# Products of 64 rows on two row tiles in the last 16 units of a three-stage kernel

## The chip, the cores and the metric

The kernel runs on one core of a Trainium2 chip. The metric is the device time of one execution in microseconds (us). The engines are TensorE (PE; its weight loads are listed apart, as PEld), VectorE (DVE), ScalarE (ACT), GpSimd (POOL) and the DMA queues, of which SyncE (SP) issues nearly all.

## What is computed

Three stages follow one another over 8192 tokens of 192 channels: a causal convolution of 7 taps, and two expansions to 2048 features and back. The first has a rational function between its products, the second a squared ReLU.

```python
out = np.einsum('hk,bskhg->bshg', w, x_unf)      # 7 taps, weights after a softmax

h = x @ w_in                                      # layer 1: 192 -> 2048
P = a[0] + a[1] * h + a[2] * h2 + a[3] * h3
Q = 1.0 + np.abs(b[0]) * np.abs(h) + np.abs(b[1]) * h2
g = P / (Q + 1e-06)
x = g @ w_out                                     # 2048 -> 192

h = x @ w_in                                      # layer 2: 192 -> 2048
r = np.maximum(h, 0.0)
g = s * (r * r) + b
out = g @ w_out                                   # 2048 -> 192
```

## The kernel before

The tokens are cut into 16 tiles of 512. The 2048 features are 16 blocks of 128, and a unit is two blocks of one tile, so there are 128 units, 8 to a tile. Every engine runs its own instruction stream over units `n` in order; streams meet only at semaphores. A loop holds tiles 2 to 13. Tiles 0 and 1, tiles 14 and 15 (units 112 to 127) and two tiles' worth of steps behind them are written out, so that `n` is a plain integer there. Layer 2 works on unit `m = n - 10` while layer 1 works on unit `n`.

In each unit TensorE issues four groups, in this order:

- the first product of layer 1 (L403 to L410), ten matmuls of 512 columns with type float32r: for each of the two blocks (`half`), the high and the low part of `x` by the high weights, the high part by the low weights, and two products with the 64 remaining channels. The tail tile `x_tail` holds the high part of those 64 channels in one half of its rows and the low part in the other; `w1_tail_hi` and `w1_tail_lo` hold their 64 rows twice. Block 0 goes to one PSUM bank of `h1`, block 1 to the other. The last matmul raises `h1_ready`.
- the second product of layer 2 for unit `m - 1` (`second_product_2`, L450 to L469): 8 float32 matmuls of 192 columns, each of which TensorE carries out as two weight loads and two matmuls (16 records in the trace), into two banks of `o2`. Where it is the tile's last (`k == UNITS - 1`) the order is by bank.
- the first product of layer 2 for unit `m` (L430 to L448), again ten matmuls of 512 columns, into the two banks of `h2`. For the first unit of a tile it waits for the parts of its input as they come: `x2_hi_ready`, `x2_lo_ready`, and the tail's two.
- the second product of layer 1 for unit `n - 2` (`second_product_1`, L412 to L428), ten matmuls of 512 columns. Six wait for `gh_ready` (ScalarE), four for `gl_ready` (GpSimd).

All matmuls use all 128 rows of the array. Each has its own weight load. `h1` has a single buffer: the first product of layer 1 waits for `t3_done` of the unit before (L539), which VectorE raises at L887 after ScalarE's L667 and L668 and its own L881 and L884. ScalarE's further steps are L672 to L721. VectorE's for the quotient are L905 to L911, and GpSimd makes the low part of `g` at L394. At step `j == 2` of a tile the results `o1` and `o1_tail` are split into the input of layer 2 (ACT L686 and L688, DVE L838 to L851).

Of the kernel before, what the change touches and what calls it, by code (L numbers as in the profile page):

```python
# [5 lines left out]
P = 128  # L6
TOK = 512
# [18 lines left out]
def conv_rational_relu2_kernel(nc, x_main, x_tail, weight, w_in1, w_out1, a, b, w_in2, w_out2, s, b2, out):  # L26
# [4 lines left out]
    D, FF = w_in1.shape  # L31
    TAIL = D - P
    FT = FF // P
    UNITS = FT // 2
# [3 lines left out]
    NU = TILES * UNITS  # L38
# [5 lines left out]
    OUT2_LAG = 1  # L44
# [31 lines left out]
    with ExitStack() as ctx:  # L76
# [6 lines left out]
        def sem(name):  # L83
            return ctx.enter_context(nc.semaphore(name))
# [3 lines left out]
        w1_hi = sb("w1_hi", [P, FF], F32R)  # L88
        w1_lo = sb("w1_lo", [P, FF], F32R)
        w1_tail_hi = sb("w1_tail_hi", [P, FF], F32R)  # L90
        w1_tail_lo = sb("w1_tail_lo", [P, FF], F32R)
# [103 lines left out]
        x2_lo_ready, x2_sum_ready = sem("x2_lo_ready"), sem("x2_sum_ready")  # L195
        x2_tail_hi_ready, x2_tail_lo_ready = sem("x2_tail_hi_ready"), sem("x2_tail_lo_ready")
        y_ready_out = sem("y_ready_out")

# [18 lines left out]
        def in_h2(n):  # L219

            return isinstance(n, int) and n < SKEW and n % 2 == 1
# [13 lines left out]
        def late_exponential(n):  # L235

            return not isinstance(n, int) or n > SKEW

        def is_end(n):
            return isinstance(n, int) and n == NU  # L240
# [159 lines left out]
        def _(pe):  # L400
            def first_product_of_layer_1(h, k, x_hi, x_lo, x_tail):

                for half in range(2):  # L403
                    c = slice((2 * k + half) * P, (2 * k + half + 1) * P)
                    pe.matmul(h[:, half, :], w1_hi[:, c], x_hi[:, :], start=True, stop=False)  # L405
                    pe.matmul(h[:, half, :], w1_hi[:, c], x_lo[:, :], start=False, stop=False)  # L406
                    pe.matmul(h[:, half, :], w1_lo[:, c], x_hi[:, :], start=False, stop=False)  # L407
                    pe.matmul(h[:, half, :], w1_tail_hi[:, c], x_tail[:, :], start=False, stop=False)  # L408
                    last = pe.matmul(h[:, half, :], w1_tail_lo[:, c], x_tail[:, :], start=False, stop=True)  # L409
                last.then_inc(h1_ready, 1)  # L410

            def second_product_1(n, k, buf):  # L412
                pe.wait_ge(gh_ready, counted(n - OUT1_LAG + 1))
                for half in range(2):
                    f = 2 * k + half
                    c = slice(half * TOK, (half + 1) * TOK)
                    tail = v1_tail[:, f].rearrange("p a b -> p (a b)")
                    pe.matmul(o1[:, :], v1_hi[:, f, :], gh[:, buf, c], start=(f == 0), stop=False)  # L418
                    pe.matmul(o1[:, :], v1_lo[:, f, :], gh[:, buf, c], start=False, stop=False)  # L419
                    pe.matmul(o1_tail[:, :], tail, gh[:, buf, c], start=(f == 0), stop=False)  # L420
                pe.wait_ge(gl_ready, counted(n - OUT1_LAG + 1))
                for half in range(2):
                    f = 2 * k + half
                    c = slice(half * TOK, (half + 1) * TOK)
                    tail = v1_tail[:, f].rearrange("p a b -> p (a b)")
                    pe.matmul(o1[:, :], v1_hi[:, f, :], gl[:, buf, c], start=False, stop=(f == FT - 1))  # L426
                    last = pe.matmul(o1_tail[:, :], tail, gl[:, buf, c], start=False, stop=(f == FT - 1))  # L427
                last.then_inc(out1_done, 1)  # L428
# [21 lines left out]
            def second_product_2(k, buf):  # L450
                def product(half, c):
                    f = 2 * k + half
                    g = g2[buf][:, half * TOK + c * P:half * TOK + (c + 1) * P]
                    return pe.matmul(o2[:, c // 2, c % 2, 0:D], g, v2[:, f, :],  # L454
                                     start=(f == 0 and c % 2 == 0), stop=(f == FT - 1), skip_group_check=True)

                if k == UNITS - 1:

                    for bank in range(2):
                        for half in range(2):  # L460
                            for c in (2 * bank, 2 * bank + 1):
                                last = product(half, c)
                        if bank == 0:
                            last.then_inc(out2_half_done, 1)
                else:
                    for half in range(2):
                        for c in range(SUB):
                            last = product(half, c)
                last.then_inc(out2_done, 1)  # L469
# [57 lines left out]
            def product_of_layer_1(n, j, t, parity):  # L527

                if j == 0:
                    pe.wait_ge(x1_hi_ready, counted((t + 1) * 2))  # L530
                    pe.wait_ge(x1_lo_ready, counted((t + 1) * 2))
                if first(t) and j in (1, 2, 4, 6):

                    high, low = {1: (2, 4), 2: (4, 6), 4: (10, 9), 6: (10, 10)}[j]
                    pe.wait_ge(w_hi_ready, high)
                    pe.wait_ge(w_lo_ready, low)

                two_buffers = isinstance(n, int) and n <= SKEW
                pe.wait_ge(t3_done, counted(n - 1 if two_buffers else n))  # L539
                first_product_of_layer_1(h2 if in_h2(n) else h1, j, x1_hi[parity], x1_lo[parity], x1_tail[parity])  # L540

            def second_product_of_layer_1(n, j, t):
                k = (j - OUT1_LAG) % UNITS
# [8 lines left out]
            def second_product_of_layer_2(t, j, m, k2):  # L552

                if unit(m - OUT2_LAG):
                    k = (k2 - OUT2_LAG) % UNITS
                    if k == 0:

                        tk = t + (j - SKEW - OUT2_LAG) // UNITS
                        pe.wait_ge(y_ready_out, counted(tk * 2))
                        pe.wait_ge(conv_copied, 4)  # L560
                        pe.wait_ge(v2_loaded, 16)
                    pe.wait_ge(g2_ready, counted(m - OUT2_LAG + 1))
                    second_product_2(k, (j - OUT2_LAG) % 2)

            def phase(n0, t, i, parity):
                for j in range(UNITS):
                    n, m = n0 + j, n0 + (j - SKEW)
                    k2 = (j - SKEW) % UNITS
                    t2 = t + (j - SKEW) // UNITS

                    early = isinstance(n, int) and n < SKEW
                    if unit(n) and not (isinstance(n, int) and n <= SKEW):
                        product_of_layer_1(n, j, t, parity)
                    if early and n == 0:
                        first_product_of_first_unit()
                    if early:
                        product_of_layer_1(n + 1, (n + 1) % UNITS, (n + 1) // UNITS, (n + 1) // UNITS % 2)

                    if tile(t):
                        second_product_of_layer_2(t, j, m, k2)  # L580
                    if j == 3 and first(t):
                        pe.wait_ge(ones_ready, 1)
                        pe.wait_ge(v2_loaded, 16)
                        for f in range(FT):
                            last = pe.matmul(o2[:, 0, 0, 0:D], ones, v2[:, f, :], start=(f == 0),
                                             stop=(f == FT - 1))
                        last.then_inc(colsum_ready, 1)
                    if early:
                        conv_of_unit(n)
                    if unit(m):  # L590
                        if k2 == 0:
                            pe.wait_ge(w_hi_ready, 13)
                            pe.wait_ge(w_lo_ready, 14)
                        if isinstance(m, int) and m == UNITS // 2:

                            pe.wait_ge(w_hi_ready, 14)
                            pe.wait_ge(w_lo_ready, 18)
                        pe.wait_ge(u_ready, counted(m))
                        if in_h2(n - 1):
                            pe.wait_ge(t3_done, n)  # L600
                        x2p = (parity + (j - SKEW) // UNITS) % 2
                        first_product_of_layer_2(k2, x2p, t2)

                    ends_layer_1 = not tile(t) and j == OUT1_LAG - 1
                    if not tile(t) and not ends_layer_1:
                        second_product_of_layer_2(t, j, m, k2)
                    if unit(n - OUT1_LAG):
                        second_product_of_layer_1(n, j, t)
                    if ends_layer_1:
                        second_product_of_layer_2(t, j, m, k2)  # L610
# [353 lines left out]
```

## Time and profile before

| | |
|---|---|
| median of the runs | 1266.53 us (2 runs, 1266.32 to 1266.73) |
| profiled execution, its own time | 1267.56 us |
| its span, first to last instruction | 1265.7 us |
| TensorE, matmuls | 1250.9 us busy, 99% of the span, 6018 records |
| TensorE, weight loads | 1078.0 us busy, 6018 records |
| VectorE | 1119.9 us |
| ScalarE | 1073.1 us |
| GpSimd | 331.4 us |
| mean granted TensorE clock | 0.997 of full speed |

The rows quoted further on have the forms of the page and of the trace's views. In the timeline a row is start, duration (both us), engine, line of the kernel, operation, output and inputs, and how often in a row; square brackets hold the idle time before it and what ended it. A matmul's duration in the trace is a modelled latency: matmuls overlap, and the time that one adds is the distance from one start to the next.

### The profile page before, as it was taken

The numbers are of one execution on the slowest core, as the hardware profiler recorded it, in microseconds if no ns is written. First come the engines' busy times: TensorE is split into PE (matmuls) and PEld (weight loads), VectorE is DVE, ScalarE is ACT, GpSimd is POOL, SyncE is SP. The second block draws the span as 40 slices with busy tenths as digits, with TensorE's granted clock in tenths as the row PEclk, the third lists the DMA queues.
The fourth block names the chain that finished last, engine by engine and source line by source line (L and its number), as shares of the span: only waits on it lengthen the run. The fifth ranks groups of instructions, "written<-read, shape, count | busy, mean of one in ns | idle before, by whom it ended". The sixth has DMA issues, their size and how long they took to land.

```text
span 1265.7 us, 16270 instructions
## 1 busy us (share of the span) xinstructions
PE 1250.9 (99%) x6018; PEld 1078.0 (85%) x6018; DVE 1119.9 (88%) x1031; ACT 1073.1 (85%) x1091; POOL 331.4 (26%) x153
## 2 busy tenths in 40 slices
PE   7999999999999999999999999999999999999999
PEld 5767888888888888888888888888888888888888
DVE  7997999998999989998999989999899998888740
ACT  6898888988989888888888889898898888888853
POOL 3443222322222222223223222222232232222210
PEclk8999999999999999999999999999999999999999
DMA  7100000010000100000000100001000000000000
GB/s 223 61 10 17 1 13 1 1 39 0 12 0 12 25 0 12 0 12 25 11 1 0 38 0 12 0 0 38 0 12 0 12 0 1 13 1 13 1 13 13
DMA packets 14748, 20.39 MB, mean 16 GB/s; under 512 B 1792, under 2 KB 9984, under 8 KB 14592
## 3 DMA queue, kind: packets, MB, share of 16 engines
q1 hardware_dynamic: 14576, 20.01, 5.4%
q8 instruction: 18, 0.29, 0.1%
q14 instruction: 10, 0.08, 0.0%
q10 hardware_dynamic: 144, 0.01, 0.0%
HBM read 13.72 MB, written 6.29 MB: 16 GB/s over the span
## 4 chain that ended last, share of the span: by engine, by line
PE 90%; DVE 6%; issue 1%; DMA 1%; ACT 1%; SPq 1%; POOL 0%; DVEq 0%; ACTq 0%
PE o L454 26%; PE h L436 5%; PE h L437 5%; PE h L441 4%; PE h L446 4%; PE h L447 4%; PE o L426 4%; PE h L405 4%; PE h L409 4%; PE o_tail L427 4%; PE h L407 4%; PE h L406 4%; PE h L408 4%; PE o_tail L420 4%; PE o L419 4%; PE o L418 4%
## 5 line engine op out<-in xcount | busy, mean ns | idle before, releaser
L394 POOL TENSOR_TENSOR gl<-work,gh 128x1024 fp32r<-128x1024 f32 x128 | 309.5, 2418 | 830.0 <-ACT gh L677 822.6
L454 PE MATMUL o<-v,work 128*128 128x192 f32 x2048 | 353.3, 326 | 0.9 <-issue 0.9
L454 PEld LDWEIGHTS o<-v,work 128*128 128x128 f32 x2048 | 339.1, 190 | 11.1 <-issue 1.3
L667 ACT ACTIVATE work<-h,coef 128x1024 f32<-128x1024 f32 x128 | 154.3, 1205 | 135.1 <-PE h L409 134.3
L881 DVE SCALAR_TENSOR_TENSOR work<-work,coef,h 128x1024 f32<-128x1024 f32 x128 | 163.8, 1280 | 74.8 <-ACT work L668 72.4
L911 DVE SCALAR_TENSOR_TENSOR work<-work,coef 128x1024 f32<-128x1024 f32 x128 | 164.5, 1285 | 4.5
L887 DVE SCALAR_TENSOR_TENSOR work<-work,coef,h 128x1024 f32<-128x1024 f32 x128 | 164.0, 1281 | 4.5
L905 DVE SCALAR_TENSOR_TENSOR work<-work,coef 128x1024 f32<-128x1024 f32 x128 | 164.1, 1282 | 0.0
L907 DVE SCALAR_TENSOR_TENSOR work<-work 128x1024 f32<-128x1024 f32 x128 | 159.0, 1242 | 4.4
L884 DVE TENSOR_TENSOR work<-work,h 128x1024 f32<-128x1024 f32 x128 | 155.4, 1214 | 0.0
L710 ACT ACTIVATE work<-h 128x1024 f32<-128x1024 f32 x128 | 130.3, 1018 | 23.9 <-PE h L447 23.8
L721 ACT ACTIVATE work<-work,coef 128x1024 f32<-128x1024 f32 x128 | 145.6, 1137 | 0.0
L668 ACT ACTIVATE work<-h,coef 128x1024 f32<-128x1024 f32 x128 | 141.3, 1104 | 0.0
L677 ACT CAST gh<-work 128x1024 fp32r<-128x1024 f32 x128 | 133.9, 1046 | 8.5 <-DVE work L911 8.3
L713 ACT ACTIVATE work<-work 128x1024 f32<-128x1024 f32 x128 | 136.0, 1063 | 4.5
L706 ACT ACTIVATE work<-work 128x1024 f32<-128x1024 f32 x128 | 134.8, 1053 | 2.9 <-DVE work L881 2.8
L672 ACT ACTIVATE work<-work 128x1024 f32<-128x1024 f32 x128 | 136.5, 1066 | 0.1
L436 PE MATMUL h<-x_hi,w_hi 128*128 128x512 f32 x256 | 117.4, 459 | 2.0 <-ACT x_hi L686 2.0
L405 PE MATMUL h<-x_hi,w_hi 128*128 128x512 f32 x254 | 99.9, 393 | 4.1 <-ACT w_tail_hi L624 4.0
L418 PE MATMUL o<-gh,v_hi 128*128 128x512 f32 x256 | 102.8, 402 | 0.0
L426 PE MATMUL o<-gl,v_hi 128*128 128x512 f32 x256 | 100.0, 391 | 0.9 <-POOL gl L394 0.8
L446 PE MATMUL h<-x_tail,w_tail_hi 128*128 128x512 f32 x256 | 99.7, 389 | 0.9 <-DVE x_tail L851 0.9
(101 smaller groups left out, 2015.3 us busy)
## 6 DMA issues: line engine op xcount, KB each, us to landing
out_dram<-y_out SPq DMA_DIRECT2D x32, 192.0 KB, 2.0
xt<-in_x_main_dram SPq DMA_DIRECT2D x7, 518.0 KB, 5.0
xt_tail<-in_x_tail_dram SPq DMA_DIRECT2D x8, 259.0 KB, 5.3
work<-in_moe_w_out_dram SPq DMA_DIRECT2D x2, 768.0 KB, 8.6
v<-in_moe_w_out_dram SPq DMA_DIRECT2D x1, 1536.0 KB, 6.2
raw_w_tail_late<-in_moe_w_in_dram SPq DMA_DIRECT2D x4, 256.0 KB, 7.1
work<-in_moe_w_in_dram SPq DMA_DIRECT2D x2, 512.0 KB, 5.7
xt<-in_x_main_dram SPq DMA_DIRECT2D x2, 259.0 KB, 7.6
```

What stands on the lines that cost most here:

```text
L394: nc.gpsimd.tensor_tensor(gl[:, j % 2, :], r_buf[j % 2], gh[:, j % 2, :].bitcast(F32), ALU.subtract).then_inc(gl_ready, 1)
L418: pe.matmul(o1[:, :], v1_hi[:, f, :], gh[:, buf, c], start=(f == 0), stop=False)
L426: pe.matmul(o1[:, :], v1_hi[:, f, :], gl[:, buf, c], start=False, stop=(f == FT - 1))
L436: pe.matmul(h2[:, half, :], w2_hi[:, c[half]], x2_hi[x2p][:, :], start=True, stop=False)
L454: return pe.matmul(o2[:, c // 2, c % 2, 0:D], g, v2[:, f, :], start=(f == 0 and c % 2 == 0), stop=(f == FT - 1), skip_group_check=True)
L667: nc.scalar.activation(t_of_n, h_flat, ACT.Identity, bias=a2, scale=a3).then_inc(t_ready, 1)
L881: nc.vector.scalar_tensor_tensor(q_buf[buf], w_of_n, b0_abs, h_flat, ALU.add, ALU.mult).then_inc(z_done, 1)
L884: nc.vector.tensor_tensor(t_of_n, t_of_n, h_flat, ALU.mult).then_inc(t2_done, 1)
L887: nc.vector.scalar_tensor_tensor(num_buf[buf], t_of_n, a1, h_flat, ALU.add, ALU.mult).then_inc(t3_done, 1)
L905: nc.vector.scalar_tensor_tensor(q, q, one_eps, r, ALU.add, ALU.mult).then_inc(e_done, 1)
L907: nc.vector.scalar_tensor_tensor(r, q, 2.0, r, ALU.subtract, ALU.mult, reverse0=True).then_inc(r1_done, 1)
L911: nc.vector.scalar_tensor_tensor(r, num, a0, r, ALU.add, ALU.mult).then_inc(g_ready, 1)
```

## The change

The diff adds three predicates. In units 112 to 127 (`rows_1`) the first product of layer 1, and in units `n` = 116 to 127 (`rows_2`) the first product of layer 2, is made by `by_rows`. In units 120 to 127 (`rows_3`), except where `k == UNITS - 1`, the second product of layer 2 is made by `second_product_2_by_rows`.

`by_rows` cuts each matmul into one over rows 0 to 63 (`LOWER`) and one over rows 64 to 127 (`UPPER`). It goes in two turns: in the first, block 0 takes the lower rows and block 1 the upper rows, alternating; in the second it is the other way round. Between the turns TensorE waits for its own matmuls of the first turn (`turned`), since both row tiles would otherwise write one bank. Of the product with `w_tail_lo` only the rows `high` are made, those that hold the high part of `x`; the product of two low parts falls away. `second_product_2_by_rows` does the same with the two banks of `o2`.

```diff
+        def rows_1(n):
+            return isinstance(n, int) and NU - 2 * UNITS <= n < NU
+
+        def rows_2(n):
+            return rows_1(n) and n >= NU - 2 * UNITS + UNITS // 2
+
+        def rows_3(n):
+            return rows_1(n) and n >= NU - UNITS
...
+            LOWER, UPPER = slice(0, P // 2), slice(P // 2, P)
+            turns = [0]
+
+            def turn_over():
+
+                turns[0] += 2
+                pe.wait_ge(turned, turns[0])
+
+            def by_rows(h, k, products, tail_low, high, done):
+
+                c = [slice((2 * k + half) * P, (2 * k + half + 1) * P) for half in range(2)]
+                for turn in range(2):
+                    for weights, x, ready in products:
+                        if turn == 0 and ready is not None:
+                            pe.wait_ge(*ready)
+                        for half in range(2):
+                            rows = (LOWER, UPPER)[(half + turn) % 2]
+                            last = pe.matmul(h[:, half, :], weights[rows, c[half]], x[rows, :],
+                                             start=turn == 0 and weights is products[0][0] and x is products[0][1],
+                                             stop=turn == 1 and weights is products[-1][0] and rows != high)
+                            if turn == 0 and weights is products[-1][0] and rows != high:
+                                last.then_inc(turned, 1)
+                    weights, x = tail_low
+                    half = turn if high == LOWER else 1 - turn
+                    last = pe.matmul(h[:, half, :], weights[high, c[half]], x[high, :], start=False, stop=turn == 1)
+                    if turn == 0:
+                        last.then_inc(turned, 1)
+                        turn_over()
+                last.then_inc(done, 1)
+
+            def first_product_of_layer_1_by_rows(h, k, x_hi, x_lo, x_tail, high):
+                by_rows(h, k, ((w1_hi, x_hi, None), (w1_hi, x_lo, None), (w1_lo, x_hi, None), (w1_tail_hi, x_tail, None)),
+                        (w1_tail_lo, x_tail), high, h1_ready)
+
+            def first_product_of_layer_2_by_rows(k, x2p, t2):
+                of_x = [(x2_hi_ready, t2 + 1), (x2_lo_ready, t2 + 1), (x2_tail_lo_ready, t2 + 1)] if k == 0 else [None] * 3
+                by_rows(h2, k, ((w2_hi, x2_hi[x2p], of_x[0]), (w2_lo, x2_hi[x2p], None), (w2_hi, x2_lo[x2p], of_x[1]),
+                                (w2_tail_hi, x2_tail[x2p], of_x[2])), (w2_tail_lo, x2_tail[x2p]), LOWER, h2_ready)
+
+            def second_product_2_by_rows(k, buf):
+                for turn in range(2):
+                    for half in range(2):
+                        f = 2 * k + half
+                        for c in range(2):
+                            for bank in range(2):
+                                rows = (LOWER, UPPER)[(bank + turn) % 2]
+                                col = half * TOK + (2 * bank + c) * P
+                                last = pe.matmul(o2[:, bank, c, 0:D], g2[buf][rows, col:col + P], v2[rows, f, :],
+                                                 start=(f == 0 and c == 0 and turn == 0), stop=(f == FT - 1 and turn == 1),
+                                                 skip_group_check=True)
+                                if turn == 0 and half == 1 and c == 1:
+                                    last.then_inc(turned, 1)
+                    if turn == 0:
+                        turn_over()
+                last.then_inc(out2_done, 1)
...
+                if rows_1(n):
+                    first_product_of_layer_1_by_rows(h1, j, x1_hi[parity], x1_lo[parity], x1_tail[parity],
+                                                     tail_rows[parity])
...
+                    if isinstance(t, int) and rows_3(t * UNITS + j) and k != UNITS - 1:
+                        second_product_2_by_rows(k, (j - OUT2_LAG) % 2)
...
+                        if rows_2(n):
+                            first_product_of_layer_2_by_rows(k2, x2p, t2)
```

## Rows read from the trace of the kernel before

**Rows 1.** The page, engines' busy time, and granted clock in 40 slices
```profile
PE 1250.9 (99%) x6018; PEld 1078.0 (85%) x6018; DVE 1119.9 (88%) x1031; ACT 1073.1 (85%) x1091; POOL 331.4 (26%) x153
...
PEclk8999999999999999999999999999999999999999
```
**Rows 2.** Busy time by stretch: matmuls, loads, DVE, ACT, POOL, clock, DMA
```profile
1054.20:1091.80 37.60, 37.60 (x186) 32.85 (x185) 34.93 (x35) 33.31 (x35) 9.69 (x4) 1.00 0.04 12
1167.00:1204.70 37.70, 37.70 (x186) 32.98 (x185) 29.65 (x25) 32.32 (x33) 9.69 (x4) 1.00 0.00 0
1204.70:1235.00 30.30, 29.36 (x148) 25.40 (x148) 12.41 (x12) 15.68 (x17) 4.78 (x2) 1.00 0.04 14
```
**Rows 3.** Timeline of unit 118, TensorE and who frees h1
```profile
1110.61 0.39 PE L405 MATMUL h<-x_hi,w_hi 128*128 128x512 f32 x1
1110.61 0.19 PEld L406 LDWEIGHTS h<-x_lo,w_hi 128*128 128x128 f32 x1
...
1112.65 0.39 PE L409 MATMUL h<-x_tail,w_tail_lo 128*128 128x512 f32 x1
1112.65 2.69 PEld L454 LDWEIGHTS o<-v,work 128*128 128x128 f32 x16
1112.88 2.76 PE L454 MATMUL o<-v,work 128*128 128x192 f32 x16
1113.13 1.20 ACT L667 ACTIVATE work<-h,coef 128x1024 f32<-128x1024 f32 x1 [1.31 <-PE h L409]
...
1115.47 0.19 PEld L437 LDWEIGHTS h<-x_hi,w_lo 128*128 128x128 f32 x1
...
1117.75 0.39 PE L418 MATMUL o<-gh,v_hi 128*128 128x512 f32 x1
1117.89 1.28 DVE L887 SCALAR_TENSOR_TENSOR work<-work,coef,h 128x1024 f32<-128x1024 f32 x1
...
1120.02 0.39 PE L405 MATMUL h<-x_hi,w_hi 128*128 128x512 f32 x1
```
**Rows 4.** Timeline where TensorE waits for ScalarE, behind unit 127
```profile
1213.66 1.05 ACT L677 CAST gh<-work 128x1024 fp32r<-128x1024 f32 x1 [2.89 <-DVE work L911]
...
1214.40 0.39 PE L447 MATMUL h<-x_tail,w_tail_lo 128*128 128x512 f32 x1
1214.76 0.19 PEld L418 LDWEIGHTS o<-gh,v_hi 128*128 128x128 f32 x1 [0.39 <-ACT gh L677]
1214.76 0.50 PE L418 MATMUL o<-gh,v_hi 128*128 128x512 f32 x1
...
1214.87 0.19 PEld L419 LDWEIGHTS o<-gh,v_lo 128*128 128x128 f32 x1
1215.09 0.40 PE L419 MATMUL o<-gh,v_lo 128*128 128x512 f32 x1
```
**Rows 5.** Timeline of unit 122, where layer 2 takes a new tile
```profile
1152.87 0.69 DVE L851 TENSOR_TENSOR x_tail<-x_sum,x_tail 64x512 fp32r<-64x512 f32 x1
...
1152.99 0.53 PE L436 MATMUL h<-x_hi,w_hi 128*128 128x512 f32 x1
1153.13 0.19 PEld L437 LDWEIGHTS h<-x_hi,w_lo 128*128 128x128 f32 x1
```
**Rows 6.** Timeline, TensorE's other waits for layer 1's last units
```profile
1211.28 0.19 PEld L426 LDWEIGHTS o<-gl,v_hi 128*128 128x128 f32 x1 [0.56 <-POOL gl L394]
...
1217.22 0.19 PEld L426 LDWEIGHTS o<-gl,v_hi 128*128 128x128 f32 x1 [1.23 <-POOL gl L394]
```

More of the change, by code:

```diff
@@ L197, in conv_rational_relu2_kernel @@
         y_ready_out = sem("y_ready_out")
+        turned = sem("turned")
         W2_HALF = [slice(0, FF // 2), slice(FF // 2, FF)]
@@ L539, in product_of_layer_1 @@
                 pe.wait_ge(t3_done, counted(n - 1 if two_buffers else n))
-                first_product_of_layer_1(h2 if in_h2(n) else h1, j, x1_hi[parity], x1_lo[parity], x1_tail[parity])
+                if rows_1(n):
+                    first_product_of_layer_1_by_rows(h1, j, x1_hi[parity], x1_lo[parity], x1_tail[parity],
+                                                     tail_rows[parity])
+                else:
+                    first_product_of_layer_1(h2 if in_h2(n) else h1, j, x1_hi[parity], x1_lo[parity], x1_tail[parity])
             def second_product_of_layer_1(n, j, t):
@@ L562, in second_product_of_layer_2 @@
                     pe.wait_ge(g2_ready, counted(m - OUT2_LAG + 1))
-                    second_product_2(k, (j - OUT2_LAG) % 2)
+                    if isinstance(t, int) and rows_3(t * UNITS + j) and k != UNITS - 1:
+                        second_product_2_by_rows(k, (j - OUT2_LAG) % 2)
+                    else:
+                        second_product_2(k, (j - OUT2_LAG) % 2)
             def phase(n0, t, i, parity):
@@ L601, in phase @@
                         x2p = (parity + (j - SKEW) // UNITS) % 2
-                        first_product_of_layer_2(k2, x2p, t2)
+                        if rows_2(n):
+                            first_product_of_layer_2_by_rows(k2, x2p, t2)
+                        else:
+                            first_product_of_layer_2(k2, x2p, t2)
                     ends_layer_1 = not tile(t) and j == OUT1_LAG - 1
```

## The prediction

> **What bounds the kernel now.** I read the page first, for which engine fills the span. Matmuls are busy 1250.9 of 1265.7 us, and the granted clock stays at its upper level in 39 of 40 slices [rows 1]. The busy time by stretch says whether this holds where the change works. In the four units from 1054.20 and in the four up to 1204.70 TensorE is busy in every microsecond, and only the stretch behind them (1204.70 to 1235.00) has 0.94 us of gaps [rows 2]. The timeline of one unit then gives the price of each instruction. From one L405 to the next unit's is 1120.02 - 1110.61 = 9.41 us [rows 3]. The ten products of 512 columns from L418 at 1117.75 to 1120.02 take 2.27 us, 0.227 each. The 16 records of L454 run from 1112.88 to the start of the next stream (when the load of L437 begins, 1115.47), 2.59 us or 0.162 each. 30 x 0.227 + 16 x 0.162 = 9.40 us, so a unit is its matmuls and nothing else: what TensorE gains or loses in units 112 to 127 is a gain or loss of the whole, nearly one to one.
>
> How much it could gain before another engine stops it: `h1` is free when L887 ends, 1117.89 + 1.28 = 1119.17, and the next L405 starts at 1120.02 [rows 3]. Slack exists, but it is 0.6 to 0.85 us a unit, and a slower TensorE widens it.
>
> **The streams: nothing removed.** Ten full matmuls become 18 half ones, which looks like nine. But a turn has five half products on the row tile that `high` names and four on the other. The wait between the turns keeps the idle tile from going on. So the path is 2 turns x 5 streams = 10 streams of 512 columns, as before. If two row tiles do run side by side and a half-height stream takes 0.227 as a full one does, the saving is 0. A bound on the gain side is the float32 rows: 0.162 us for 192 columns in two cycles each is 0.422 ns a column-cycle, or 0.216 for 512 [rows 3]. By that rate it would be 28 products x 10 x 0.011 = 3.1 us. I take 0.
>
> **The wait between turns: added, 35 times.** There are 28 products by rows (16 of layer 1 and 12 of layer 2) and 7 second products of layer 2 (units 120 to 127 without 122). The wait can't be answered before the last matmul has written, and the next load stands behind the wait. Nothing else is in that engine's queue, so nothing hides it. Three pieces. A matmul's record lasts 0.39 us where the next one starts 0.23 after it, so 0.16 is not covered [rows 3]. From ScalarE's end at 1213.66 + 1.05 = 1214.71 to the load that waited for it (1214.76) is 0.05. That load keeps the matmul waiting until 1214.87, 0.11 more [rows 4]. 0.16 + 0.05 + 0.11 = 0.32, and 35 x 0.32 = 11.2 us. Lower bound 0.16 (the load passes the wait): 5.6. Upper bound: from a last matmul's modelled end, 1112.65 + 0.39, to the start of the ScalarE instruction that waited for it, 1113.13, are 0.09 [rows 3]; in place of 0.05 that gives 0.36, 12.6 us.
>
> **The second tile starts late: 28 times.** In each turn the second tile's load can begin only when the first one's is done, 0.11 later [rows 4]. In one of a product's two turns `high` is the second tile, and its five streams end 0.11 after 5 x 0.227. 28 x 0.11 = 3.1 us; the lower bound is 0, if both load at once. Further on, two loads take 0.22 in a pair's 0.227, which just fits.
>
> **The second product of layer 2: loads become the limit.** Its weights are `g2`, new in every matmul. 16 records become 32, each with a load. At 0.11 a load that is 3.52 us where the streams need 16 x 0.162 = 2.59: +0.93 in each of 7 units, 6.5 us. In the rows every load begins as the matmul before it starts [rows 3]. If that holds over two tiles too, the order A, A, B, B of the two passes gives 2 x (0.162 + 0.11) = 0.544 for four records, 8 x 0.544 = 4.35 us, +1.76 a unit and 12.3 us in all. The other end is 0 (two tiles load side by side). I take 6.5, which rests on the measured load alone.
>
> **Changing between 128 and 64 rows.** No row of before shows such a change. There are 42: two in each of units 112 to 115, four in 116 to 119, two in the seven units where all three groups are by rows, four in unit 122 (8 + 16 + 14 + 4). The lower end is 0: a load of float32 weights into a float32r stretch starts on time, at 1112.65 [rows 3]. The upper end is a full drain and a load behind it, 0.16 + 0.11 = 0.27, or 11.3 us. I take the drain alone, 0.16 x 42 = 6.7 us. The Trainium skill has a rule that speaks against this change ("TensorEngine Tiling (Array Packing)", Key Properties): changing the tiling mode drains the engine. With the rule the 6.7 stands or becomes 11.3; without it the term is 0. No row here shows it.
>
> **What takes some back, what costs nothing.** Behind unit 127 TensorE waits 0.56, 0.39 and 1.23 us for layer 1's last elementwise chain [rows 4, 6]. In unit 127 the slower groups after its layer 1 product add about 1.25 (second product) + 0.6 (first product of layer 2), and that chain runs on meanwhile: -1.5 us, between -2.2 and 0. The reordered waits of unit 122 cost nothing. The tail is ready at 1152.87 + 0.69 = 1153.56, while the stream starts at 1153.13 and comes to the tail after three pairs, at 1153.81 [rows 5]. The `h1` loop grows with the product itself and stays under the longer unit. The 28 x 8 + 7 x 16 = 336 more matmul records and their loads are fetched beside the work.
>
> **Sum:** 11.2 + 3.1 + 6.5 + 6.7 - 1.5 = +26.0 us on the profiled 1267.6, or 1293.6. The median of the runs is 1.0 lower, so **1293 us**, +2.1%. With every term at its lower bound (5.6 - 2.2 - 3.1) it is about 0, with every term at its upper one (12.6 + 3.1 + 12.3 + 11.3) +39. With only the second products and the change of height at 0 it is 11.2 + 3.1 - 1.5 = +12.8. Own range: 1279 (+12.8) to 1306 (+39).
>
> **Rivals.**
>
> *A, no overlap.* The row tiles don't run side by side, so the change does not do what it says. 8 more streams in 28 products, 224 x 0.227 = 50.8 us, and 16 more records in 7 units, 112 x 0.162 = 18.1 us. With the turns and switches (11.2 + 6.7 - 1.5) that is +85, 1352 us. For it: no row of before shows two matmuls in the array. Against: the tiles share neither rows nor banks. The skill has a measured gain of 3.07 for four row tiles of 32 rows ("TensorE: Matmul & The Clock Gate", Measured speedup vs the span model); no run here shows it.
>
> *B, loads don't hide under a matmul of their own rows.* Each stream then costs its load as well, 0.227 + 0.11 = 0.337. A turn is 5 x 0.11 = 0.55 longer, 56 turns 30.8 us; the second products go to 16 x (0.162 + 0.11) = 4.35, +12.3. With 11.2 + 3.1 + 6.7 - 1.5 it is +63, 1329 us. The skill has the rule that loads overlap matmuls in flight only where the row group differs (same page, The mechanism). The trace speaks against it for full-height matmuls: the load of L406 begins with the matmul of L405 at 1110.61, and the next starts 0.227 later [rows 3]. It may hold for tiles.
>
> *C, not slower by what can be measured.* The two tiles load weights side by side and across a change of height, so nothing of the load side is new: stagger, second products and switches all 0. Only the turns are left, 11.2 - 1.5 = +9.7, 1276 us. It decides from where those three terms (16.3 here) fall below some 15. For it: the rows bound them below by 0. Against: the load is a single record stream at 0.11 apiece.
>
> *D, the clock.* Shorter bursts with gaps of a third of a us could let the granted clock fall to its lower level. A unit at 1.2 GHz costs nearly twice 9.4, so a few of them would be +20 us and more. Against: gaps of 0.56 and 1.23 us leave the clock at 1.00 in that stretch [rows 2, 6].
>
> **Chances.** The forecast with its own range 0.67, A 0.10, B 0.11, C 0.10, D 0.02. The range leaves out A and D and the lower part of C and takes in B: 1277 to 1330. Some 2% (25 us) is what can be told from no change, and my sum lies at that edge. Of the forecast's 0.67, 0.35 lies above it and 0.32 below. Slower by over 2%: 0.35 + 0.10 + 0.11 + 0.02 = 0.58. Within 2%: 0.32 + 0.09 = 0.41. Faster by over 2% is 0.01: the 280 streams by rows (63.6 us) would have to be 40% shorter, at no cost for the turns.
>
> **What would show it.** The new products as 64-row records, block 0 and block 1 starting 0.11 apart and each tile's next 0.227 later (right) or 0.227 and 0.454 (A), 0.337 (B). A gap of 0.55 from a turn's last start to the next turn's first matmul. The distance from L454's last record to the first half-height one near 0.33 (drain) or 0.16 (none). Second products by rows of 3.5 + 0.3 us. Units 112 to 115 at about 10.2 us, 120 to 127 at about 12. I am wrong if a tile's stream is far from 0.227, or if a change of height costs more than a turn.

## The result, and the profile after

| | before | after |
|---|---|---|
| median of the runs | 1266.53 us | 1287.85 us (2 runs, 1287.76 to 1287.93) |
| profiled execution, its span | 1267.56, 1265.7 us | 1287.76, 1285.9 us |
| matmul records | 6018 | 6354 |
| VectorE, ScalarE busy | 1119.9, 1073.1 us | 1119.8, 1074.4 us |

The changed kernel takes 1.0167 of the time before, with a 95% interval of 1.0147 to 1.0187. That is 21.3 us more by the medians and 20.2 us by the spans of the two profiles. The number foretold was 1293, the range 1277 to 1330.

In the page of the changed kernel the other engines do the same work as before [rows 1]. The granted clock (one digit a slice, in tenths) stays at its upper level from the first slice to the last:

```profile
PE 1270.8 (99%) x6354; PEld 1074.4 (84%) x6354; DVE 1119.8 (87%) x1031; ACT 1074.4 (84%) x1091; POOL 330.7 (26%) x153
...
PEclk9999999999999999999999999999999999999999
```

The 19.9 us more of matmul "busy" time are not all work, since a matmul's record is a latency. Where the time sits is seen in the timeline of the changed kernel's first unit by rows, 112 (start, duration, engine, line, operation, how many; in brackets the idle time before it and what ended it). L441 and L448 are `by_rows`, L522 is the full-height second product of layer 2:

```profile
1054.06 0.20 PEld L441 LDWEIGHTS h<-x_hi,w_lo 64*128 64x128 f32 x2
1054.29 0.40 PE L441 MATMUL h<-x_hi,w_lo 64*128 64x512 f32 x2
1054.29 0.20 PEld L441 LDWEIGHTS h<-x_tail,w_tail_hi 64*128 64x128 f32 x2
1054.52 0.40 PE L441 MATMUL h<-x_tail,w_tail_hi 64*128 64x512 f32 x2
1054.53 0.18 PEld L448 LDWEIGHTS h<-x_tail,w_tail_lo 64*128 64x128 f32 x1
1054.76 0.38 PE L448 MATMUL h<-x_tail,w_tail_lo 64*128 64x512 f32 x1
1055.20 0.19 PEld L441 LDWEIGHTS h<-x_hi,w_hi 64*128 64x128 f32 x2 [0.49 <-PE h L448]
...
1055.31 0.19 PEld L441 LDWEIGHTS h<-x_lo,w_hi 64*128 64x128 f32 x2
...
1056.24 0.39 PE L448 MATMUL h<-x_tail,w_tail_lo 64*128 64x512 f32 x1
...
1056.56 2.57 PEld L522 LDWEIGHTS o<-v,work 128*128 128x128 f32 x16 [0.37 <-issue]
```

Three things are to be read here.

- Two half-height matmuls start together: a pair is one line of 0.40 us, and the next pair starts 0.23 us after it, where full-height matmuls stand 0.227 apart [rows 3]. Their two weight loads go together too: both fit in 0.20 us, where one takes 0.19.
- The turn: the last stream of turn 1 starts at 1054.76, the next load at 1055.20 and its stream at 1055.31, where the load after it starts. That is 0.55 in place of 0.23, so the turn (the point where TensorE waits for its own matmuls) costs 0.32.
- The change of height: from the last short stream at 1056.24 to the load of the next full one at 1056.56 are 0.32, and 0.11 more to its stream. That is 0.43 in place of 0.23, so a change costs 0.20. Its releaser is "issue": the profile shows nothing that is waited for.

The change in the other direction costs as much, 1063.60 to 1063.92 to 1064.03 at the start of unit 113:

```profile
1063.60 0.39 PE L495 MATMUL o_tail<-gl,v_tail 128*128 128x512 f32 x1
...
1063.92 0.19 PEld L441 LDWEIGHTS h<-x_hi,w_hi 64*128 64x128 f32 x2 [0.35 <-issue]
...
1064.03 0.19 PEld L441 LDWEIGHTS h<-x_lo,w_hi 64*128 64x128 f32 x2
```

So unit 112 takes 1053.83 to 1064.03 between the first streams of its layer 1 products, 10.20 us against 9.41 [rows 3]: one turn (0.32), two changes (0.40), and 0.07 for streams a little further apart (four distances in 0.93 us from 1053.83, 0.233 each, in place of 0.227). In the last tile, where all three groups are by rows, a unit takes 10.93 us (1193.27 to 1204.20), and there the full-height streams of L486 to L495 stand 0.231 apart as well. Whatever spaces the streams out is therefore not the half height alone.

What TensorE's loads waited for from unit 112 on, in the changed kernel (us in total, times, longest):

```profile
PEld h L441 <- PE h L448: 13.6, 28, 0.5
PEld h L441 <- issue: 6.5, 20, 0.4
...
PEld o L486 <- issue: 4.4, 12, 0.4
PEld o L522 <- issue: 3.3, 9, 0.4
PEld o L471 <- PE o L471: 2.5, 7, 0.4
...
PEld o L494 <- POOL gl L406: 1.0, 1, 1.0
```

28 + 7 = 35 waits of TensorE for itself, as counted. Of the 42 changes of height, 41 show here as idle time ended by "issue" (20, 12 and 9); the first, into unit 112 at 1053.72, lies before this window. The last row is the wait for layer 1's chain behind unit 127, which was 2.18 us in three places before [rows 4, 6].

### The profile page after: what moved, and what is told of

Its sections match the earlier page's. It is cut to its first block, busy times and chain, and to the rows that moved or that the text cites. A ratio compares the mean times of both kernels' runs of the same rounds, so it can differ in the third digit from the quotient of the medians.

```text
span 1285.9 us, 16941 instructions
## 1 busy us (share of the span) xinstructions
PE 1270.8 (99%) x6354; PEld 1074.4 (84%) x6354; DVE 1119.8 (87%) x1031; ACT 1074.4 (84%) x1091; POOL 330.7 (26%) x153
## 4 chain that ended last, share of the span: by engine, by line
PE 90%; DVE 6%; issue 1%; DMA 1%; ACT 1%; SPq 0%; POOL 0%; DVEq 0%; ACTq 0%
PE o L522 24%; PE h L441 5%; PE o L486 4%; PE o L494 4%; PE o_tail L495 4%; PE o_tail L488 4%; PE o L487 4%; PE h L514 4%; PE h L504 4%; PE h L515 4%; PE h L505 4%; PE h L509 4%; PE h L418 4%; PE h L421 4%; PE h L420 4%; PE h L419 4%
## 5 line engine op out<-in xcount | busy, mean ns | idle before, releaser
L522 PE MATMUL o<-v,work 128*128 128x192 f32 x1936 | 335.0, 326 | 0.6 <-issue 0.6
L522 PEld LDWEIGHTS o<-v,work 128*128 128x128 f32 x1936 | 319.9, 190 | 12.9 <-issue 4.3
L504 PE MATMUL h<-x_hi,w_hi 128*128 128x512 f32 x232 | 106.5, 459 | 2.5 <-ACT x_hi L764 2.5
L486 PE MATMUL o<-gh,v_hi 128*128 128x512 f32 x256 | 104.1, 407 | 0.0
L488 PE MATMUL o_tail<-gh,v_tail 128*128 128x512 f32 x256 | 99.8, 390 | 0.0
L487 PE MATMUL o<-gh,v_lo 128*128 128x512 f32 x256 | 99.8, 390 | 0.0
```

Source lines behind the costliest of these rows:

```text
L504: pe.matmul(h2[:, half, :], w2_hi[:, c[half]], x2_hi[x2p][:, :], start=True, stop=False)
```

## The experiments

Theory T, formed on this profile: 35 turns at 0.32 us and 42 changes of height at 0.20 us make 19.6 us of the 21.3, and the streams and loads add next to nothing. Rival S: half-height matmuls side by side slow one another down. The experiments take away each cost alone, or put it alone into the kernel before. All times are beside runs of the kernel before on the same chip. Numbers in brackets behind a ratio are its 95% interval. Where two changed kernels are compared, it is by their medians; the kernel before has medians of 1266.53 to 1267.09 us from set to set, so such a difference holds to about 0.5 us.

### The turn taken away

```diff
-                            rows = (LOWER, UPPER)[(half + turn) % 2]
+                            rows = (LOWER, UPPER)[half]
...
-                    half = turn if high == LOWER else 1 - turn
+                    half = 0 if high == LOWER else 1
...
-                    if turn == 0:
-                        last.then_inc(turned, 1)
-                        turn_over()
```

(and the same in `second_product_2_by_rows`)

> The changed kernel, but in the second turn each block stays on the row tile it had in the first, so the wait between the turns falls away (the products of the other row halves are left out, and the same halves are made twice: as many matmuls, in as many streams). Theory T (the loss is 35 waits for TensorE's own matmuls at 0.32 us each and 42 changes between 128 and 64 rows at 0.20 us each, all else near 0): 11.2 us less than the changed kernel, about 1276.6 us. Rival S (half-height matmuls side by side are themselves slower, by contention of their streams or loads): stays near 1287.

Measured: 1273.92 us beside 1266.64, ratio 1.0056 (1.0040 to 1.0073), +7.3 us. The waits were worth 13.9 us here, 2.7 more than 35 x 0.32. The trace shows from where. In this kernel without waits, at the end of a second product (L466), one row tile already loads the next group's weights (L441) while the other tile is not done:

```profile
1138.07 0.19 PEld L441 LDWEIGHTS h<-x_hi,w_hi 64*128 64x128 f32 x1
1138.21 0.19 PEld L466 LDWEIGHTS o<-v,work 64*128 64x128 f32 x1
1138.23 0.19 PEld L441 LDWEIGHTS h<-x_hi,w_lo 64*128 64x128 f32 x1
1138.37 0.19 PEld L466 LDWEIGHTS o<-v,work 64*128 64x128 f32 x1
1138.46 0.18 PEld L441 LDWEIGHTS h<-x_lo,w_hi 64*128 64x128 f32 x1
```

The tile that has four streams in a turn where the other has five doesn't stand idle any more but goes ahead. A unit of the last tile takes 9.51 us here (1133.78 to 1143.29) with two changes of height in it, so by subtraction 9.11 without them, under the 9.41 of full height. Two things come together for this that only the last tile has. All three groups there are by rows, so the free tile has something to go on with. And `tail_rows` puts layer 1's extra product on the upper rows in this tile, while layer 2's is always on the lower ones, so that both tiles have 18 streams of 512 columns in a unit (both tiles' last loads start at 1140.07). In units 116 to 119 a full-height group stands between the two products, and both have their extra product on the lower rows. There a unit of this kernel takes 10.27 us (1092.58 to 1102.85): 9.41, four changes (0.80) and 0.06, and no gain. So in the last tile the turns cost their wait, and most of the only gain that the change could have had. Rival S falls: as many half-height matmuls and changes of height, and 14 us less.

### The turn alone, at full height

The kernel before, with a wait for itself in the middle of the same 35 groups:

```diff
+            def turn_over(last):
+                turns[0] += 1
+                last.then_inc(turned, 1)
+                pe.wait_ge(turned, turns[0])
...
+                    if waits and half == 0:
+                        turn_over(last)
```

> The kernel before with all products of full height, and a wait for TensorE's own matmuls put into the middle of the same 35 groups that have one in the changed kernel. T: 35 x 0.32 = +11.2 us, about 1277.5, up to 1.2 less for what is absorbed behind unit 127. Rival S: near 1266.5 to 1269. If the weight load can pass the wait: 35 x 0.21, about 1274.

Measured: 1278.09 us beside 1266.64, ratio 1.0092 (1.0075 to 1.0109), +11.5 us; T said +11.2. In this kernel's timeline (L417 is the last matmul of block 0, L413 the first of block 1) the parts are those of the prediction:

```profile
1164.19 0.39 PE L417 MATMUL h<-x_tail,w_tail_lo 128*128 128x512 f32 x1
...
1164.64 0.19 PEld L413 LDWEIGHTS h<-x_hi,w_hi 128*128 128x128 f32 x1 [0.48 <-PE h L417]
...
1164.75 0.19 PEld L414 LDWEIGHTS h<-x_lo,w_hi 128*128 128x128 f32 x1
1164.98 0.19 PEld L415 LDWEIGHTS h<-x_hi,w_lo 128*128 128x128 f32 x1
1165.22 0.19 PEld L416 LDWEIGHTS h<-x_tail,w_tail_hi 128*128 128x128 f32 x1
1165.46 0.19 PEld L417 LDWEIGHTS h<-x_tail,w_tail_lo 128*128 128x128 f32 x1
```

0.45 us from the last stream's start to the load, 0.11 to the next stream: 0.56. The wait has nothing to do with row tiles.

The last three rows show more. Behind the wait each load stands 0.23 to 0.24 us after the one before it, where 0.227 is the distance in the kernel before, and this is a kernel without one half-height matmul. A unit with a single turn takes 9.81 us here (1052.25 to 1062.06 between its first loads), which is 9.41, the turn at 0.33 and 0.07: the same 0.07 as in unit 112 of the changed kernel. So the wider distance follows an interruption of TensorE, at full height too. Over the 16 units the profiled execution is 12.5 us longer, more than T's 11.2, and 0.8 us of TensorE's waits behind unit 127 fall away (2.2 before, 1.4 here). That +11.5 lies so near T is partly because these two cancel.

### The change of height alone

The kernel before, with one or both of the last matmuls of layer 1's product cut to 64 rows in units 112 to 127 (`short` is the rows with the high part of x):

```diff
-                    last = pe.matmul(h[:, half, :], w1_tail_lo[:, c], x_tail[:, :], start=False, stop=True)
+                    r = slice(0, P) if short is None or half not in (1,) else short
+                    last = pe.matmul(h[:, half, :], w1_tail_lo[r, c], x_tail[r, :], start=False, stop=True)
```

> The kernel before, but in units 112 to 127 the last matmul of layer 1's first product uses only the 64 rows with the high part of x (the product of two low parts falls away for that block). One short matmul among full ones, 32 changes of height, no wait and no second tile. T: 32 x 0.20 = +6.4 us, about 1272.9. If a change of height costs nothing and the gap is due to the turn or to two tiles: 1266.5. If it costs a full drain and a load, 0.27 each: 1275.2.

> As the run with one short matmul, but both blocks' last matmul uses 64 rows, with full ones between: 64 changes of height. T: twice the other run's cost, +12.8 us, about 1279.3. If only a first change or one direction costs: less than twice.

Measured: 1273.11 us (ratio 1.0049, 1.0032 to 1.0066) and 1280.03 us (1.0102, 1.0085 to 1.0119) beside 1266.64, +6.5 and +13.4 us. That is 0.20 and 0.21 for each of 32 and 64 changes, in proportion, with no second tile, and with no wait between the matmuls of the product. One short matmul among full ones, in the first of the two kernels:

```profile
1163.29 0.39 PE L408 MATMUL h<-x_tail,w_tail_hi 128*128 128x512 f32 x1
1163.61 0.18 PEld L410 LDWEIGHTS h<-x_tail,w_tail_lo 64*128 64x128 f32 x1 [0.35 <-issue]
...
1164.03 0.62 PEld L455 LDWEIGHTS o<-v,work 128*128 128x128 f32 x4 [0.24 <-issue]
```

The load of the other height starts 0.32 us after the matmul before it, where a load of the same height starts with it [rows 3]. The short matmul runs from 1163.72 (0.11 behind its load), and the load back to full height starts 0.31 after that.

### Parts of the change alone

Layer 1's first product alone by rows, and layer 2's second product alone by rows (the other two conditions set to `False`):

> Only layer 1's first product is made by rows (16 units): 16 waits, 32 changes of height. T: 16 x 0.32 + 32 x 0.20 = +11.5 us, about 1278. Rival S (cost by the number of half-height matmuls, 288 of the changed kernel's 504 of 512 columns, and none of the 224 of 192): about 1276 or less, with streams over 0.227 us apart in the trace.

> Only layer 2's second product is made by rows, in 7 units: 7 waits, 14 changes of height. T with weights of two tiles loaded side by side: 7 x 0.32 + 14 x 0.20 = +5.0 us, about 1271.5. The forecast's term (loads one by one, 0.93 us a unit) would make it +11.5, about 1278.

Measured: 1279.57 us (ratio 1.0100, 1.0083 to 1.0117) and 1271.46 us (1.0036, 1.0021 to 1.0050) beside 1267.09: +12.5 and +4.4 us, where T said +11.5 and +5.0. Both values of T lie in the intervals (the ratio's, times 1267.09). The second run decides on the forecast's largest wrong term: the +11.5 that it would give is far outside. Its loads are seen to go in parallel. In this kernel a turn's 16 loads take 1.28 us, 0.08 each, where 0.11 apiece would make 1.76:

```profile
1160.75 1.28 PEld L471 LDWEIGHTS o<-v,work 64*128 64x128 f32 x16 [0.35 <-issue]
1162.42 1.28 PEld L471 LDWEIGHTS o<-v,work 64*128 64x128 f32 x16 [0.39 <-PE o L471]
1163.92 0.19 PEld L504 LDWEIGHTS h<-x_hi,w_hi 128*128 128x128 f32 x1 [0.23 <-issue]
```

### The product that was left out, put back

```diff
+                    for half in range(2):
+                        rows = (LOWER, UPPER)[(half + turn) % 2]
+                        last = pe.matmul(h[:, half, :], weights[rows, c[half]], x[rows, :], start=False, stop=turn == 1)
```

> The changed kernel with the product of two low parts made too: 20 half-height matmuls for a product in place of 18, the two more on the row tile that is otherwise idle. If the path is the fuller tile's 10 streams, as the prediction has it: the same time, 1287.8. If TensorE's time goes by the number of matmuls: 56 x 0.115 = +6.4, about 1294.

Measured: 1288.53 us beside 1267.09, ratio 1.0169 (1.0152 to 1.0186), +21.4 us; the changed kernel has +21.3. 56 more matmuls cost nothing that the times can tell, where 6.4 us were foretold for a time that goes by their number. A turn is as long as its fuller tile. The traces differ a little: a unit of the last tile is 11.03 us here (1194.17 to 1205.20) and 10.93 in the changed kernel. There the tile without the low product goes on to the second product while the other still has its L448 to do:

```profile
1195.45 0.19 PEld L448 LDWEIGHTS h<-x_tail,w_tail_lo 64*128 64x128 f32 x1
1195.45 1.62 PEld L471 LDWEIGHTS o<-v,work 64*128 64x128 f32 x16
```

So leaving the product out did save something, 0.10 us a unit, where the next group was by rows and no turn stood between.

### Other work between the turns

In seven units of the last tile (units 120 to 127 without 122) the turns of layer 2's two products are interleaved:

```diff
-                        second_product_2_by_rows(k, (j - OUT2_LAG) % 2)
+                        second_product_2_by_rows(k, (j - OUT2_LAG) % 2, (0,))
...
+                            first_product_of_layer_2_by_rows(k2, x2p, t2, (lambda: second_product_2_by_rows(
+                                k2 - 1, (j - OUT2_LAG) % 2, (1,))) if split else None)
```

> The changed kernel with other work put between the turns of layer 2's two products in the seven units where both are by rows: second product's turn 1, first product's turn 1, second's turn 2, first's turn 2. 14 of the 35 waits are then answered before TensorE comes to them. T: 14 x 0.32 = 4.5 us less than the changed kernel, about 1283.4. Rival: ScalarE's chain takes the wait's place because the second product is done 1.1 us later, and nothing is gained, 1287.8.

Measured: 1281.92 us beside 1267.09, ratio 1.0117 (1.0100 to 1.0133), +14.8 us: 5.9 less than the changed kernel's median, where T said 4.5. The 14 waits are gone (TensorE waits for itself 21 times, not 35). A unit is 10.02 us (1137.71 to 1147.73) in place of 10.93, which is 0.27 more than two waits; the free tile's going ahead, as in the first experiment, would account for it, though nothing here measures it apart.

Then layer 1's product was opened too, with turn 1 of the second product between its turns; and, as a second kernel, this in the seven units alone, with everything else at full height:

```diff
+                    first_product_of_layer_1_by_rows(h1, j, x1_hi[parity], x1_lo[parity], x1_tail[parity],
+                                                     tail_rows[parity], (lambda: second_product_of_layer_2(
+                                                         t, j, n - SKEW, k2)) if inside else None)
```

> The interleaved kernel, and layer 1's first product is opened too: layer 1 turn 1, second product turn 1, layer 1 turn 2, layer 2 turn 1, second product turn 2, layer 2 turn 2, in seven units of the last tile. No wait between turns is exposed there, and a row tile with four streams can go on into the next group. T with the idle streams recovered: 7 x (0.32 + about 0.25) = 4 us less than the interleaved kernel, about 1278. Without the recovery: 7 x 0.32 = 2.2 less, about 1279.7. Rival: layer 1's elementwise chain, which gets its input about 1 us later, becomes the limit: no gain.

> As that one, but only those seven units are by rows; units 112 to 119 and unit 122 are as in the kernel before. What is left are 14 changes of height against the recovered idle streams. T: 7 x (0.40 - 0.3 to 0.45), 0 to +0.7 us: 1266.3 to 1267.5, no worse than the kernel before and no better by more than noise. Without the recovery: 7 x 0.40 = +2.8, about 1269.4. If the elementwise chain limits: more.

Measured: 1287.77 us (ratio 1.0164, 1.0149 to 1.0180) and 1276.46 us (1.0076, 1.0063 to 1.0090) beside 1266.55. Both are misses of T, and the rival named for them holds: the first is 5.9 us slower than without the opening, the second +9.9 us where 0 to 0.7 was expected. The waits of the second kernel in the last tile:

```profile
PEld o L501 <- POOL gl L406: 7.5, 6, 1.3
PE o L501 <- POOL gl L406: 4.9, 6, 0.8
PEld o L493 <- ACT gh L767: 3.4, 6, 0.6
```

TensorE now waits for `gh` and `gl` once in each of the six units by rows that this window covers in full. `h1` was ready 1.2 us later (ScalarE's L757 starts 3.97 us into the unit, its L667 in the kernel before 2.75), and ScalarE, which takes its steps in a fixed order, made `gh` behind it. The slack was small all along: in the kernel before GpSimd's `gl` was done 0.3 us before its matmuls.

The last kernel tests this. It is the one with seven units by rows, but only two matmuls of the second product (4 records) stand between the turns of layer 1's product:

```diff
-                        second_product_2_by_rows(k, (j - OUT2_LAG) % 2, (0,))
+                        second_product_2_by_rows(k, (j - OUT2_LAG) % 2, (0,), (0,))
...
+                    if rows_3(n):
+                        second_product_2_by_rows(k2 - 1, (j - OUT2_LAG) % 2, (0,), (1, 2, 3))
```

> The kernel with seven units by rows, but between the turns of layer 1's first product stand only the first two matmuls of the second product (4 of its 16 records of that turn, 0.33 us) in place of all 16 (1.3 us); the rest follows behind layer 1's product. If the elementwise chain was the limit because layer 1's product ended 1 us later: the chain is back under TensorE's time, and a unit is 9.41 + 0.40 (changes of height) - 0.37 (idle streams recovered), so 1266.5 + 7 x 0.04, about 1267, at par with the kernel before. If the limit was something else in the interleaving (layer 2's turns, the drift of the row tiles): it stays at about 1276.

Measured: 1269.79 us (11 runs) beside 1266.80, ratio 1.0024 (1.0015 to 1.0033), +3.0 us. That is 6.7 us less than with all 16 records between the turns, so the late `h1` was the cause of most of those 9.9. It is still 3 us slower than the kernel before and not at par. The loads' waits in one unit show what is left:

```profile
1164.31 0.19 PEld L495 LDWEIGHTS o<-gh,v_hi 128*128 128x128 f32 x1 [0.36 <-issue]
1165.80 0.19 PEld L503 LDWEIGHTS o<-gl,v_hi 128*128 128x128 f32 x1 [0.27 <-POOL gl L406]
1166.93 0.19 PEld L440 LDWEIGHTS h<-x_hi,w_hi 64*128 64x128 f32 x2 [0.36 <-issue]
...
1176.75 0.18 PEld L440 LDWEIGHTS h<-x_hi,w_hi 64*128 64x128 f32 x2 [0.36 <-issue]
```

No wait of TensorE for itself is left. A unit is 9.82 us (1166.93 to 1176.75), 0.41 above full height. It holds two changes of height (0.40) and a short wait for `gl` in every unit. By this sum the idle streams recovered pay for no more than that wait and the wider distances behind the interruptions; they were not measured apart. As long as layer 1's second product is at full height, the two changes eat what the row tiles bring. A version with that product by rows as well, which would need no change inside the tile, was not tried.

## Why the prediction was right, point by point

The direction, the size and the range held: +26.0 was the sum, +21.3 came (+20.2 in the profiles). The mechanism held for the larger half, waits and changes of height with nothing to gain from the streams. For the rest it did not: 9.6 us of the sum stood on loads that wait for one another, which they do not, and some 4 us that were missing elsewhere made good part of it. That the sum missed by only 5 us is to that extent luck. Its terms fared as follows.

- **TensorE sets the pace**: right. Nothing else waited longer in a way that mattered, and the path grew by TensorE's idle time.
- **The streams, 0**: right in what decides. The pairs stand 0.23 apart, and the run with the left-out product put back has the same time. Streams further apart add about 2 us that were not foreseen: a unit is 0.07 us longer than its turns and changes in units 112 to 115, 0.14 in 116 to 119 (10.99 us, 1094.52 to 1105.51) and about 0.16 in the last tile. The run with waits at full height shows that they follow an interruption and not the half height. Why they do stays open.
- **The turns, 11.2 us**: right, with 0.32 to 0.33 each in the trace (0.37 where the second product stands alone) and +11.5 measured alone at full height, wider streams and the shorter waits behind unit 127 included.
- **The second tile's late start, 3.1 us**: wrong, it is 0. The two tiles load side by side.
- **Loads as the limit of the second product, 6.5 us**: wrong for the same reason, it is 0. The step that failed is "At 0.11 a load that is 3.52 us", which took the rate of loads on one full-height array for a limit of the whole engine. The two tiles' 16 loads of a turn take 1.28 us, and 7 units by rows cost +4.4 us in all and not +11.5.
- **The change of height, 6.7 us**: mis-sized. It is 0.20 and not 0.16 each, 42 x 0.20 = 8.4 us. The load does not wait for all of the 0.16 that is left of a matmul's record but for 0.09, and then it is not hidden, 0.11 more. By the rule in "TensorEngine Tiling (Array Packing)" of the Trainium skill (Key Properties: changing the mode drains the engine) the trace agrees: a gap of 0.43 us in place of 0.23 stands at the changes behind a 512-column stream, in both directions. The page gives no price.
- **Given back behind unit 127, 1.5 us**: 1.2 (2.18 of waits before, 1.0 after).

With these, 11.2 + 8.4 + 2 - 1.2 = 20.4 us beside the spans' 20.2. The agreement is no closer than the spans allow: the first load of unit 112 comes at 1052.25 to 1054.61 us in the profiled executions, before the edits have set in.

Of the rivals, A (no overlap) and B are refuted. B rested on a rule of the Trainium skill ("TensorE: Matmul & The Clock Gate", The mechanism), that loads overlap matmuls in flight only where the row group differs. The trace contradicts it for tiles as it did for the full array: the loads at 1054.29 start with the matmuls of the same two row groups, and the pairs stay 0.23 apart. C was half right: the loads do go side by side, but not across a change of height, and so two of its three terms fell and the third grew. D did not occur: the granted clock is 1.00 in every stretch from 1045 us on.

The chances were less good. 0.58 stood on slower by over 2%, and the time came out 1.67% longer. The two load terms, 9.6 us together, put the sum over that edge; without them it would have been +16.4. Of the signs, the turn's 0.55 and units 112 to 115 at 10.2 us came as written. From a 192-column stream of L522 to the first half-height one are 0.37 us (last start at 1110.90, load at 1111.15, stream 0.11 later) where "near 0.33 (drain)" was written. "120 to 127 at about 12" was wrong by the load terms, it is 10.9.

## What to carry to other kernels

Splitting a full-height product over two row tiles saved nothing by itself here: the time is that of the fuller tile. A product dropped from one tile counts only if that tile may run ahead into a next group that is also by rows, and, by the count of streams, if that group gives the free tile more to do than the other. What is paid is each change between 128 and 64 rows (0.20 us here, hidden by nothing) and each wait of TensorE for its own result (0.32 us), so count both before counting matmuls, and put independent work between the turns. That work delays the product that it splits; where an elementwise chain behind it has only 0.3 us of slack, insert just enough to cover the wait.

## What the runs showed of the hardware

- Two row tiles of 64 rows take float32r matmuls of 512 columns in parallel: a pair every 0.23 us, against 0.227 for one of full height. Their weight loads run in parallel as well, 16 in 1.28 us.
- The tiles are independent enough that one starts the next group while the other is still in the last: it took a unit's work in the last tile from 9.41 to about 9.11 us, changes of height apart.
- A change of height costs 0.20 to 0.21 us, in proportion over 32 and 64 changes. The load of the other height starts 0.32 us after the start of a 512-column matmul, in either direction (0.25 after a 192-column one of L522), and its own 0.11 us is not hidden.
- TensorE waiting for its own matmul costs 0.32 us more than not waiting, at full and at half height.
- Behind such a wait or a change the matmuls of 512 columns stand up to 0.24 us apart for a while in place of 0.227, at either height: 0.07 us in a unit with one wait at full height.
